# Gated attention in front of two feed-forward layers: the first two steps of each attention duo done on even and odd tokens

## The reference, cut to what matters

```python
def _attn_ref(q, k, v, f_logit):
    f = 1.0 / (1.0 + np.exp(-f_logit))
    for t in range(S):                       # S = 768, per batch (4) and head (8), D = 48
        state = f[:, :, t, :, None] * state + np.einsum('bhd,bhe->bhde', k[:, :, t], v[:, :, t])
        y[:, :, t] = np.einsum('bhd,bhde->bhe', q[:, :, t], state)

def _moe_ref(x, U, V, w_ch1, w_ch2):
    h = x.transpose(0, 2, 1) @ U @ V                      # rank 32 over the tokens
    u = x + h.transpose(0, 2, 1)
    return u + np.maximum(u @ w_ch1, 0.0) @ w_ch2         # 384 -> 1536 -> 384

def _moe2_ref(x, w_in, conv_w, w_out):
    h = np.maximum(x @ w_in, 0.0)                         # 384 -> 1024
    conv_out = sum(conv_w[k] * shifted(h, k - 1) for k in range(3))
    return (h / (1.0 + np.exp(-conv_out))) @ w_out        # gate = sigmoid(conv_out)
```

## Time and profile before

| | us |
|---|---|
| median of 3 runs (lowest, highest) | 741.04 (740.38, 743.48) |
| the profiled execution, whole | 744.54 |
| its span, first to last instruction | 742.0 |
| PE busy in the span | 706.2 (95%) |
| DVE, ACT, POOL busy | 440.7, 246.5, 288.9 |

### The profile page before, as it was taken

The page is one execution under the profiler, slowest core; times in us unless marked ns, Lnnn a source line. Parts: engine busy times, 40 slices in busy tenths (PEclk is TensorE's granted clock), DMA queues, the critical chain, the costliest instruction groups (busy, mean ns, idle before and its releaser), DMA issues.

```text
span 742.0 us, 23831 instructions
## 1 busy us (share of the span) xinstructions
PE 706.2 (95%) x10748; PEld 665.3 (90%) x10748; DVE 440.7 (59%) x705; ACT 246.5 (33%) x505; POOL 288.9 (39%) x262
## 2 busy tenths in 40 slices
PE   2788989999999999999999999999999999999997
PEld 2777789989999899999999989999999989999997
DVE  5896384483798555355498755364489832121874
ACT  1034434333246432213245531313234542121553
POOL 3762498593363134053254215145055211030432
PEclk9999999999999999999999999999999999999999
DMA  9341253331101110201200200121000000000000
GB/s 162 102 119 42 76 162 104 93 97 42 48 2 55 44 56 6 62 23 24 66 1 23 76 34 25 28 61 23 24 2 2 34 33 1 1 1 0 1 33 32
DMA packets 24293, 33.75 MB, mean 45 GB/s; under 512 B 5152, under 2 KB 17184, under 8 KB 24192
## 3 DMA queue, kind: packets, MB, share of 16 engines
q1 hardware_dynamic: 23184, 30.46, 15.4%
q10 hardware_dynamic: 1008, 1.77, 1.2%
HBM read 27.50 MB, written 4.72 MB: 43 GB/s over the span
## 4 chain that ended last, share of the span: by engine, by line
PE 73%; DVE 16%; issue 4%; ACT 2%; POOL 2%; DMA 1%; SPq 0%; POOLq 0%; ACTq 0%; DVEq 0%
PE acc L690 8%; PE hb L671 7%; PE hb L672 6%; PE hb L673 6%; PE acc L691 6%; PE acc L692 6%; PE att L556 6%; DVE q_t L955 4%; DVE conv L1046 4%; PE att L602 3%; PE acc L726 3%; PE acc L728 3%; PE acc L727 3%; PE hb L639 2%; PE hb L707 2%
## 5 line engine op out<-in xcount | busy, mean ns | idle before, releaser
L1016 DVE SCALAR_TENSOR_TENSOR r_lo<-hb,r_hi 128x386 fp32r<-128x386 f32 (+1 forms) x96 | 53.5, 557 | 193.6 <-ACT r_hi L846 193.6
L846 ACT ACTIVATE r_hi<-hb 128x386 fp32r<-128x386 f32 (+1 forms) x96 | 47.2, 492 | 257.7 <-PE hb L673 257.7
L1126 POOL TENSOR_TENSOR r_lo<-conv,r_hi 128x384 fp32r<-128x384 f32 x64 | 61.8, 965 | 168.1 <-ACT r_hi L861 168.1
L690 PE MATMUL acc<-r_hi,w_ch_hi 128*128 128x386 f32 (+1 forms) x288 | 103.7, 360 | 0.0
L1089 POOL TENSOR_TENSOR k_t<-k_t,blocks 112x512 f32<-112x512 f32 x60 | 81.2, 1355 | 56.2 <-PE att L556 46.2
L671 PE MATMUL hb<-u_hi,w_ch_hi 128*128 128x386 f32 (+1 forms) x288 | 98.5, 342 | 0.2 <-DVE r_lo L1016 0.2
L672 PE MATMUL hb<-u_hi,w_ch_lo 128*128 128x386 f32 (+1 forms) x288 | 97.6, 339 | 0.0
L691 PE MATMUL acc<-r_hi,w_ch_lo 128*128 128x386 f32 (+1 forms) x288 | 97.3, 338 | 0.0
L692 PE MATMUL acc<-r_lo,w_ch_hi 128*128 128x386 f32 (+1 forms) x288 | 97.0, 337 | 0.0
L673 PE MATMUL hb<-u_lo,w_ch_hi 128*128 128x386 f32 (+1 forms) x288 | 96.9, 336 | 0.0
L556 PEld LDWEIGHTS att<-q_t,k_t 48*64 48x64 f32 (+3 forms) x3840 | 59.5, 134 | 29.5 <-issue 27.8
(11 more groups left out here) (133 smaller groups left out, 1339.7 us busy)
## 6 DMA issues: line engine op xcount, KB each, us to landing
v_p<-in_vn_dram SPq DMA_DIRECT2D x12, 384.0 KB, 3.9
out_dram<-ostage SPq DMA_DIRECT2D x24, 192.0 KB, 2.0
q_t<-in_qT_dram SPq DMA_DIRECT2D x21, 192.0 KB, 3.6
k_t<-in_kT_dram SPq DMA_DIRECT2D x21, 192.0 KB, 3.5
gates<-in_fT_dram SPq DMA_DIRECT2D x21, 192.0 KB, 3.5
ostage<-in_w_ch_dram SPq DMA_DIRECT2D x14, 192.0 KB, 2.6
conv<-in_w_ch_dram SPq DMA_DIRECT2D x10, 192.0 KB, 2.8
ostage<-in_w_out_dram SPq DMA_DIRECT2D x5, 192.0 KB, 3.3
```

Of the source, the lines that this page charges most:

```text
L690: pe.matmul(o, wh[:, j, ws], r_hi[:, s, 0:width], start=(j == 0), stop=False)
```

## The change

DIAG becomes EVEN: the even tokens' raw q (32 columns) against raw k. DVE then multiplies only the even tokens' q by their gates, while POOL, already at this step, multiplies the even tokens' k by the gate of the odd token behind them and makes the pairs' products. Level 0 then multiplies the odd tokens' raw q with that k into the other 32 columns of the same PSUM block: this gives both the odd diagonal and the pair scores. It waits for k alone. One masked copy of 128x1024 (`first_mask`, even tokens first, then odd) takes both steps' scores; the odd q is multiplied by the pair's product in one go. Beside this: `consts()` stands before the first loads on SP; the state update of a duo is cut in two, chunks 0 and 1 at U, the others one slot later (task `states`; at the start both stand together); `second1` and `second2` do their six matmuls on `r_hi` first and wait for `r_lo` only then; in the out task each accumulator is copied as soon as it is done (`tile_done`), and the very last half batch's middle one is copied by DVE.

```diff
-DIAG, T, U, Y = -1, LEVELS, LEVELS + 1, LEVELS + 2
+EVEN, T, U, Y = -1, LEVELS, LEVELS + 1, LEVELS + 2
...
+            order += [("states", n) for n, st in at.get(s - 1, []) if st == U]
             for n, st in at.get(s, []):
                 order.append(("att", n, st))
...
+            consts()
             for task in ORDER:
...
@@ tensor: attention
-                if st == DIAG:
+                if st == EVEN:
...
-                                mm = pe.matmul(banks[o:o + C, par, g * C:(g + 1) * C], k[rows, first:first + C],
-                                               q[rows, first:first + C], start=True, stop=True, skip_group_check=True)
+                                even = split_blocks(q[rows, first:first + C], 1)[:, :, 0, :]
+                                mm = pe.matmul(banks[o:o + C, par, g * C:g * C + 32], k[rows, first:first + C],
+                                               even, start=True, stop=True, skip_group_check=True)
...
-                    pe.wait_ge(q_ready, levels(n, st - 1))
+                    pe.wait_ge(k_ready, gated(n, max(st - 1, 0)))
                     if st > 0:
-                        pe.wait_ge(k_ready, gated(n, st - 1))
-                    if by_vector(n, st - 1):
-                        pe.wait_ge(level_taken, taken(n, st - 1))
-                    else:
-                        pe.wait_ge(quarters_taken, quarters(n))
-                    left = C - c if st >= 3 else C
+                        pe.wait_ge(q_ready, levels(n, st - 1))
+                        if by_vector(n, st - 1):
+                            pe.wait_ge(level_taken, taken(n, st - 1))
+                        else:
+                            pe.wait_ge(quarters_taken, quarters(n))
+                    left, half = C - c if st >= 3 else C, 32 if st == 0 else 0
...
@@ tensor: second2 (second1 likewise)
-                pe.wait_ge(g_lo_ready, 2 * N2 * b + q + 1)
+                pe.wait_ge(g_hi_ready, 2 * N2 * b + q + 1)
...
                     pe.matmul(o, r_hi[:, s, ts], wl[:, j, :], start=False, stop=False)
+                pe.wait_ge(g_lo_ready, 2 * N2 * b + q + 1)
+                for t in range(3):
+                    o, ts = acc[:, t, 0:DM], slice(t * P, (t + 1) * P)
                     mm = pe.matmul(o, r_lo[:, s, ts], wh[:, j, :], start=False, stop=(j == N2 - 1))
+                    if j == N2 - 1 and t < 2:
+                        mm.then_inc(tile_done, 1)
                 mm.then_inc(second_done, 1)
...
@@ vector: take_scores and attention
-                if st == DIAG:
+                if st == 0:
                     nc.vector.copy_predicated(
-                        sc[:].rearrange("p (g t) -> p g t", t=C),
-                        diag_mask[:].rearrange("p (o t) -> p o t", o=1).broadcast_to([P, BLOCKS, C]),
-                        from_psum).then_inc(level_taken, 1)
+                        sc[:].rearrange("p (g n two) -> p g two n", g=BLOCKS, two=2),
+                        first_mask[:].rearrange("p (o two n) -> p o two n", o=1, two=2).broadcast_to([P, BLOCKS, 2, 32]),
+                        from_psum.rearrange("p g (two n) -> p g two n", two=2)).then_inc(level_taken, 1)
...
-                    nc.vector.tensor_tensor(q, q, gates[i][0:PR, :], ALU.mult).then_inc(q_ready, 1)
+                    even = split_blocks(q, 1)[:, :, 0, :]
+                    nc.vector.tensor_tensor(even, even, split_blocks(gates[i][0:PR, :], 1)[:, :, 0, :],
+                                            ALU.mult).then_inc(q_ready, 1)
+                elif st == 0:
+
+                    dve.wait_ge(pairs_ready, paired(n, 0))
+                    dve.wait_ge(level_done, levels(n, 0))
+                    odd = split_blocks(q, 1)[:, :, 1, :]
+                    nc.vector.tensor_tensor(odd, odd, products(gates[i], blocks[i], 1).rearrange("p (n o) -> p n o", o=1),
+                                            ALU.mult).then_inc(q_ready, 1)
```

More of the change, by code:

```diff
@@ L37 @@
 QUADRANTS = [(par, ch) for par in range(2) for ch in range(2)]
-DIAG, T, U, Y = -1, LEVELS, LEVELS + 1, LEVELS + 2
-STEPS = list(range(DIAG, Y + 1))
+EVEN, T, U, Y = -1, LEVELS, LEVELS + 1, LEVELS + 2
+STEPS = list(range(EVEN, Y + 1))
 PAD = 2
@@ L464, in _ @@
                     if n == DUOS - 1:
-                        sp.wait_ge(level_done, levels(0, DIAG))
+                        sp.wait_ge(level_done, levels(0, EVEN))
                     load_q(n)
@@ L555, in attention @@
                                 moving = split_blocks(q[rows, first:first + C], c)[:, :, 1, :]
-                                mm = pe.matmul(banks[o:o + left, par, g * C:g * C + 32], k[rows, first:first + left],
+                                mm = pe.matmul(banks[o:o + left, par, g * C + half:g * C + half + 32], k[rows, first:first + left],
                                                moving, start=True, stop=True, skip_group_check=True)
@@ L753, in load @@
                 if n == DUOS - 1:
-                    act.wait_ge(level_done, levels(0, DIAG))
+                    act.wait_ge(level_done, levels(0, EVEN))
                 act.wait_ge(cleared_q, n + 1)
@@ L872, in out_task @@
             def out_task(b, part):
-                act.wait_ge(second_done, slots(b, 2 * N1 + N2 * (part + 1) - 1))
                 if b == 0 and part == 0:
@@ L936, in take_scores, with update_states @@
                     from_psum[:, :, 0:32].rearrange("p g (n c) -> p g n c", c=c)).then_inc(level_taken, 1)
+            def update_states(n, ccs):
+                i, j = set_of(n), n % DUOS
+                banks = duo_banks[i]
+                for cc in ccs:
+                    u, ch = cc // 2, cc % 2
+                    old, new = (4 * j + cc) % STATES, (4 * j + cc + 1) % STATES
+                    sums = banks[0:PR, ch, u * PAIRS * D:(u + 1) * PAIRS * D].rearrange("p (r e) -> p r e", e=D)
+                    if cc == 0 and j > 0:
+                        dve.wait_ge(state_ready, states(n, 0) - 1)
+                    if cc == 0 and j == 0:
+                        dve.wait_ge(update_done, updates(n))
+                        nc.vector.tensor_copy(state[0:PR, new], sums).then_inc(state_ready, 1)
+                        continue
+                    whole = products(gates[i], blocks[i], LEVELS).rearrange(
+                        "p (u r two o) -> p u r two o", u=2, two=2, o=1)[:, u, :, ch, :]
+                    if cc > 0:
+                        dve.wait_ge(state_ready, states(n, cc) - 1)
+                    nc.vector.tensor_tensor(state[0:PR, new], state[0:PR, old], whole.broadcast_to([PR, PAIRS, D]),
+                                            ALU.mult).then_inc(decay_done, 1)
+                    if cc == 0:
+                        dve.wait_ge(update_done, updates(n))
+                    dve.wait_ge(decay_done, states(n, cc) - (n // DUOS + 1))
+                    nc.vector.tensor_tensor(state[0:PR, new], state[0:PR, new], sums, ALU.add).then_inc(state_ready, 1)
             def attention(n, st):
@@ L1053, in _ @@
                     attention(*task[1:])
+                elif kind == "states":
+                    update_states(task[1], range(2, chunks(task[1])))
                 elif kind == "rank":
@@ L1065, in _ @@
                     mul2(task[1], 2 * N2 - 1)
+                elif kind == "out" and last_out(task[1], task[2], 1):
+                    dve.wait_ge(tile_done, 4 * B)
+                    dve.wait_ge(stored, 16 * (6 * B - 3))
+                    nc.vector.tensor_copy(ostage[:, 1, :], acc[:, 1, 0:DM]).then_inc(last_copied, 1)
         @block.gpsimd
```

80 lines of the change are left out of this document (41 added, 39 removed).

## The result

The changed kernel is slower: median 750.84 us (747.91 to 751.6) against 740.71 us for the kernel before, a ratio of 1.0113 with the interval 1.0077 to 1.0149. Its profiled execution took 747.91 us with a span of 746.1; it is the fastest of its four runs, while the profiled one of before (744.54, span 742.0) lay above all four of its own (739.78 to 743.48). So the two profiles show 4.1 us of a difference of 10.

The account below looks back on a forecast made before the run. PE's own work and its few waits bound the kernel; start -0.2, level 1 +1.9, r_hi matmuls first -0.3 and end -1.3 sum to +0.1 us, forecasting 741.1 us, range 735.4 to 744.8.

Parts of the forecast that it names:

- The masked copy: DVE's one copy of 1024 at stride two per duo would take 2.57 us, ends 1.31 and 3.2.
- duos 6 and 9: Level 1 waits for DVE's q and masked copy and comes 1.1 us later in each.
- Rival 1: Masked copy runs at the contiguous rate, 1.31 us, so level 1 waits less; 738.7 us, 17%.
- Duo 3: Level 1 comes 1.1 us later, but level 2 at 103.45 instead of 103.76: a gain of 0.3.
- Duo 4: One of six duos where q and copy end before level 1 is due: hidden, by 0.08 us.
- rival 3: Copy outlasts the slot from level 0 to level 1, or POOL delays DVE's q; 746.1 us, 10%.
- The start: Level 1 could begin 0.85 us sooner, but PE's code pause still ends at 24.24; gain 0.2 us.
- if the pause ends by 22: Sign of being wrong: PE's code pause in its fourth task, expected to end near 24.2, ends by 22.
- Rival 2: PE's code packet follows its request and comes earlier, 3.5 us kept to the end; 737.8 us, 15%.
- Hi first: Less waiting for r_lo in three batches, gain 0.3 us; reservation: the same matmul also waits for ACT's accumulator copies.
- States in two slots: Lets r_lo through earlier on DVE; the later half is covered by 9 to 18 matmuls; 0 us.
- The end: Last nine matmuls follow 0.79 us sooner and the last copies and issues finish earlier; gain 1.3 us, ends 0.8 and 1.6.

Follow-up runs that it names:

- second profile: The changed kernel profiled once more, nothing edited; span 748.6 us, median 750.52 us, ratio 1.0092 to the kernel before.
- split: Changed kernel with two masked copies of 512, after EVEN and after level 0, in the nine duos beside the feed-forward; 746.42 us, ratio 1.0056 to before.
- rest: Kernel before with all of the change but the attention steps; 740.31 us, ratio 0.9966 to before.
- copyfirst: Changed kernel with contiguous masked copy, made ahead of the odd q's multiplication in all duos but the first; 739.58 us, ratio 0.9965 to before.
- copyfirst2: The same kernel as copyfirst run once more, unedited; 741.33 us, ratio 0.9971 to before.
- firstlate: The copyfirst kernel with the constants loaded behind duo 0's q, k and f; 742.59 us, ratio 0.9995 to before.
- hybrid: Changed kernel with even and odd steps and contiguous copy in duos 0 to 2 alone, other duos' attention as before; 740.03 us, ratio 0.9969 to before.
- with the pause: Kernel before with an unused DVE row sum ahead of level 0's q multiplication in the nine duos beside the feed-forward; 749.06 us, ratio 1.0098.

## Why the prediction was wrong

- **The masked copy**: 2.57 us forecast from the stride, 2.42 to 2.48 measured. Right, and with it duos 6 and 9: level 1 waits 1.55 for DVE's copy, 1.1 later in each, as worked out. Rival 1 (1.31 us at this stride) is out; it took another layout to get 1.31.
- **Duo 3: the step that failed most.** The sum had a gain of 0.3, it was a loss of 4.1 (17.52 us from the first step to level 2, instead of 13.40). I took q at its 0.69 us, since POOL's pieces had hit a later q before. But moving POOL's k one step ahead also moved the pieces up: they now stand beside the odd q, which took 2.77, and behind it comes the long copy. The waits moved from 0.43 + 1.50 to 3.62, and half clock followed. The row of 3.47 us was the warning; I used it only for a rival.
- **Duo 4**: called hidden by 0.08 us. Its q took 1.85 beside POOL's pieces, and level 1 waited 1.13. Duos 5, 7, 8, 10 and 11, where no pieces are left, were hidden, as worked out. So rival 3's cause was right, POOL holding DVE's q off, but of its six duos only this one waited; it had 10%, and its 746.1 us were too low.
- **The clock was no term at all.** Half clock cost 1.6 us behind duo 6 (level 1 to level 2 in 5.97 instead of 4.41 us) and over 1 in duo 3. Nothing in this stage of the trace of before showed it, with a clock of 1.00 behind waits of up to 1.5 us; a range that ended at 744.8 had no room for it.
- **The start**: gain 0.2 forecast, 1.6 in the second profile (4.3 in the first, 2.7 of them by an earlier full rate). The pause ended at 20.81, so the prediction's own sign of being wrong ("if the pause ends by 22") came true. That the packet comes at the end of the loads held; that this end stays, since the bytes are the same, was the wrong half: they ended some 3 us sooner. Nor did the constants delay duo 0's loads: EVEN began at 8.38 as DIAG had. Rival 2 had the pause's end about right (3.4 us earlier), but for the wrong reason, and most of it did not last: all the pauses that are put down to "issue" come to 8.8 and 7.6 us in the two profiles, 6.5 before, where I had put the later ones as unchanged.
- **Hi first**: 0.3 forecast, nothing came. At the start of the second half batch, in three of the batches, PE waited 0.35 and 0.32 us for POOL's r_lo and 0.40 for ACT's copies before; after, it waits three times for ACT's copies, 1.2 us in all against 1.1. The reservation stood in the text and should have set the term to 0.
- **States in two slots**: 0 forecast, since Y stands two slots behind U; PE now waits for DVE's state update three times, 0.5 us in all.
- **The end**: 1.3 forecast, 1.1 measured. The last rows:

```profile
740.77 0.34 PE L742 MATMUL acc<-w_out_hi,r_hi 128*128 128x384 f32 x1
...
742.25 0.86 ACT L905 COPY ostage<-acc 128x384 f32<-128x384 f32 x2 [1.79 <-PE acc L747]
742.37 0.56 DVE L1117 COPY ostage<-acc 128x384 f32<-128x384 f32 x1 [2.46 <-PE acc L747]
742.75 1.30 SPq L526 DMA_DIRECT2D out_dram<-ostage  x3
```

  From the last nine matmuls' start to the end of the span it was 5.67 us before (742.0 - 736.33) and is 5.33. And they follow the matmuls ahead at once, where they had begun 0.97 us after the last one's start instead of 0.18, so those 0.79 were right.

A smaller slip: the stages of the earlier trace rows are 87% of the span (647.4 of 742.0), not 88%. With the copy's stride as it is, and read afterwards from the second profile, the sum is: start -1.6, duo 3 +4.1, duo 4 +1.2, duo 6 +2.7, duo 9 +1.1, the rest to the end -0.9: 6.6 us, which is the span of the second profile less that of before (748.6 - 742.0). The medians differ by more, 7.6 us in its group.

## What to carry to other kernels

A copy's price hangs on the layout it writes as much as on its size: look for rows of the same operation at the same stride before merging two copies, and let the engine for which the stride is free do the interleaving (here PE, full as it is: it wrote at stride two in the same 1.14 us). Where work is moved a step ahead on one engine, follow what stands behind it there too, and price a two-input multiplication at its slow rows (2.77 and 1.85 us, not 0.69) wherever the neighbour's large operations now stand beside it. A wait between two steps on the full engine counts, not the total of the engine that causes it: with the same copying on DVE, split got some 40% of the loss back.

## What the runs showed of the hardware

- Half clock behind PE's waits. In duo 3: 6.8 us after waits of 2.8 to 3.6 us (five profiles), 3.4 us after 2.5 (two), and after waits of 1.25 to 1.55 us either 3.4 us (rest, copyfirst, copyfirst2, firstlate) or none (before, hybrid). At duo 6: 3.4 us after 1.55 in four profiles of four, none after 1.75 with the pause; at duo 9 none after 1.55 or 1.75.
- In the first 59 us PE's small matmuls take as long as at half clock (1.93 us for the 64 records that take 1.14 later), while the granted clock reads 1.00 in all profiles; between 59 and 80 us it reads half for a while in six of the thirteen. The full rate begins at times that differ by 9 us between two executions of one kernel (69.5 and 78.4), and duo 3's first step came 2.7 us sooner in the one that had it first.
- A write to PSUM at stride two by PE's matmuls of 32 columns costs nothing (1.14 us for 64 records); a write to SBUF at stride two by DVE's masked copy nearly doubles its time (2.46 us instead of 1.31).
